# Decayed attention and two expanding layers on one core: four edits to the opening and to the order of the second products

## The reference, cut to what matters

```python
for t in range(S):                       # attention: 4 batches, 8 heads, 768 tokens, 48 wide
    state = alpha[:, :, t, :, None] * state + np.einsum('bhd,bhe->bhde', k[:, :, t], v[:, :, t])
    y[:, :, t] = np.einsum('bhd,bhde->bhe', q[:, :, t], state)
x = y.transpose(0, 2, 1, 3).reshape(3072, 384)
h = x @ w_in;   g = h * np.tanh(softplus(h));  x = g @ w_out      # first layer, 384 -> 2048 -> 384
h = x @ w_in2;  g = h * np.cos(h);             out = g @ w_out2   # second layer, the same shape
```

## Time and profile before

| | us |
|---|---|
| three runs | 902.21, 902.39, 904.98 |
| median | 902.39 |
| the profiled execution | 904.68 |
| its span, first to last instruction | 902.6 |
| PE busy (matmuls) | 887.0 (98% of the span) |
| DVE, ACT, POOL busy | 402.9, 410.4, 361.2 |
| mean granted TensorE clock | 0.994 |

### The profile page before, as it was taken

One profiled execution on the slowest core, in us unless ns is written; L12 is line 12 of the kernel. 1 busy time (PEld: TensorE's weight loads), 2 busy tenths in 40 slices (PEclk: granted clock), 3 DMA queues, 4 the chain that ended last, 5 costly groups with the idle time before them and its releaser, 6 DMA issues.

```text
span 902.6 us, 13960 instructions
## 1 busy us (share of the span) xinstructions
PE 887.0 (98%) x5536; PEld 729.0 (81%) x5536; DVE 402.9 (45%) x625; ACT 410.4 (45%) x702; POOL 361.2 (40%) x281
## 2 busy tenths in 40 slices
PE   7799999999999999999999999999999999999997
PEld 6588888888888888888888788888888888888885
DVE  8664432222223322210021666665666575666653
ACT  3344332223223232322354756565665565665654
POOL 3576344444443345442256333332323232323332
PEclk9899999999999999999999999999999999999999
DMA  8535321112112311210032300200200200200000
GB/s 218 167 98 161 98 74 39 39 39 75 39 39 54 95 41 39 74 30 1 36 123 91 101 2 1 70 1 1 70 1 1 71 0 1 71 1 1 35 1 36
DMA packets 17153, 48.13 MB, mean 53 GB/s; under 512 B 2752, under 2 KB 2752, under 8 KB 17088
## 3 DMA queue, kind: packets, MB, share of 16 engines
q1 hardware_dynamic: 17088, 47.23, 17.8%
HBM read 37.79 MB, written 9.44 MB: 52 GB/s over the span
## 4 chain that ended last, share of the span: by engine, by line
PE 52%; issue 29%; POOL 14%; DVE 2%; DMA 1%; ACT 1%; POOLq 0%; ACTq 0%; SPq 0%; DVEq 0%
PE bank L413 22%; PE bank L433 22%; POOL g_lo L762 14%; PE bank L341 3%; PE bank L362 2%; PE bank L369 1%; PE bank L374 1%; PE bank L335 1%; PE bank L385 1%; DMA shared<-mid 1%; DVE growth L604 0%; DVE suffix L593 0%; DMA shared<-aqk_in 0%; DVE w_lo L651 0%; DVE probs L625 0%
## 5 line engine op out<-in xcount | busy, mean ns | idle before, releaser
L762 POOL TENSOR_TENSOR g_lo<-g,g_hi 128x512 fp32r<-128x512 f32 x192 | 263.3, 1372 | 484.3 <-ACT g_hi L506 484.3
L433 PE MATMUL bank<-g_hi,w_hi 128*128 128x512 f32 x576 | 226.9, 394 | 0.3 <-DVE x_out L664 0.3
L433 PE MATMUL bank<-g_lo,w_hi 128*128 128x512 f32 x576 | 224.6, 390 | 0.6 <-POOL g_lo L762 0.6
L433 PE MATMUL bank<-g_hi,w_lo 128*128 128x512 f32 x576 | 224.3, 389 | 0.0
L506 ACT ACTIVATE g_hi<-g 128x512 fp32r<-128x512 f32 x192 | 120.6, 628 | 145.1 <-PE bank L433 143.5
L413 PE MATMUL bank<-x_hi,w_hi 128*128 128x512 f32 x576 | 163.0, 391 | 4.7 <-POOL w_lo L754 3.6
L413 PE MATMUL bank<-x_hi,w_lo 128*128 128x512 f32 x576 | 162.4, 390 | 0.0
L413 PE MATMUL bank<-x_lo,w_hi 128*128 128x512 f32 x576 | 162.4, 390 | 0.0
L413 PEld LDWEIGHTS bank<-x_hi,w_hi 128*128 128x128 f32 x576 | 108.1, 188 | 28.4 <-issue 4.0
L433 PEld LDWEIGHTS bank<-g_hi,w_hi 128*128 128x128 f32 x576 | 108.1, 188 | 25.2 <-DVE x_out L664 0.7
L433 PEld LDWEIGHTS bank<-g_lo,w_hi 128*128 128x128 f32 x576 | 108.1, 188 | 24.7 <-POOL g_lo L762 1.9
(11 more groups left out here) (69 smaller groups left out, 594.8 us busy)
## 6 DMA issues: line engine op xcount, KB each, us to landing
w_raw<-w_in SPq DMA_DIRECT2D x32, 384.0 KB, 3.5
shared<-aqk_in SPq DMA_DIRECT2D x44, 192.0 KB, 3.6
v_sb<-v_in SPq DMA_DIRECT2D x24, 256.0 KB, 4.5
shared<-aqk_in SPq DMA_DIRECT2D x48, 96.8 KB, 3.9
mid<-x_out SPq DMA_DIRECT2D x6, 768.0 KB, 5.1
shared<-mid SPq DMA_DIRECT2D x6, 768.0 KB, 5.7
out<-x_out SPq DMA_DIRECT2D x5, 768.0 KB, 4.0
out<-x_out SPq DMA_DIRECT2D x3, 256.0 KB, 2.4
```

The source lines that it names most:

```text
L433: mm = nc.tensor.matmul(acc[m][:, :], wp[:, f, cols], gp[:, tile % GB, :], start=(f == 0 and n == 0), stop=(f == FT - 1 and n == 2))
L762: nc.gpsimd.tensor_tensor(g_lo[:, tile % GB, :], g[:, tile % GB, :], g_hi[:, tile % GB, :].bitcast(F32), ALU.subtract).then_inc(glo_ready, 1)
```

## The change

Five things are changed. ACT and POOL split piece 2 earlier. The masked scores of chunks 1 and 3 go to a buffer of their own (the unused third parts of `x_out` and `g`), and `mask` of chunks 2 and 3 waits for one `values` less. `add_state` of chunks 1 to 3 moves from DVE's opening into step 2, behind `mask(4)`. Second products of slices above 0 take the three matmuls with `g_lo` last; for the very last tile each bank reports by itself when it is done (`last_done`), and ACT takes the last tile's absolute value (`fold`) ahead of `g_part` of the tile before it. Seven `warm` matmuls are added.

```diff
+        def probs_of(c, i):
+            if c in (1, 3):
+                return (x_out[:, 2, :], g[:, 2, :])[i].rearrange("p (a t) -> p a t", a=PAIRS)
+            return probs[:, i, :, :]
...
-                for m in range(KT):
-                    if f == 0 and j > 0:
+                parts = ((w_hi, g_hi), (w_lo, g_hi), (w_hi, g_lo))
+                order = [(m, n) for m in range(KT) for n in range(3)]
+                if f > 0:
+                    order = [(m, n) for m in range(KT) for n in range(2)] + [(m, 2) for m in range(KT)]
+                for i, (m, n) in enumerate(order):
+                    if f == 0 and j > 0 and n == 0:
...
-                        if m == 0 and gp is g_lo:
-                            pe.wait_ge(glo_ready, tile + 1)
...
+                    if (m, n) == (0, 2):
+                        pe.wait_ge(glo_ready, tile + 1)
+                    wp, gp = parts[n]
...
+                    if tile == 2 * TILES - 1 and n == 2:
+                        mm.then_inc(last_done, 1)
+                    elif i == len(order) - 1:
+                        mm.then_inc(out_done, 1)
...
             scores(0)
-            warm(4)
+            warm(8)
             scores(1)
+            warm(3)
             values(0, -1)
...
             def take_acc(j):
-                act.wait_ge(out_done, FT * (j + 1))
+                last = j == 2 * BLOCKS - 1
+                if not last:
+                    act.wait_ge(out_done, FT * (j + 1))
                 if j > 0:
                     act.wait_ge(stored, 16 * j)
                 for m in (0, 2):
+                    if last:
+                        act.wait_ge(last_done, m + 1)
...
+                if s == 2 * TILES:
+                    fold(s - 1)
                 if alive(s - 2) and s - 2 >= TILES:
                     g_part(s - 2)
                 if alive(s - 1) and s - 1 >= TILES:
+                    if s < 2 * TILES:
+                        fold(s - 1)
                     cosine(s - 1)
...
             split_w(1)
+            split_w(2)
             keep_x_hi(3)
-            split_w(2)
             split_w(3)
...
             def mask(c):
-                if c >= 1:
-                    dve.wait_ge(y_done, c)
+                if c >= 2:
+                    dve.wait_ge(y_done, c if c >= BATCH else c - 1)
...
                     mask(c)
+                if s == 2:
+                    for c in range(1, BATCH):
+                        add_state(c)
...
-            for c in range(BATCH):
-                add_state(c)
+            add_state(0)
             split_w(3)
...
             split_w(0)
+            split_w(2)
             prepare(4)
-            split_w(2)
```

More of the change, by code:

```diff
@@ L206, in program @@
         out_done = sem("out_done")
+        last_done = sem("last_done")
         acc_act = sem("acc_act")
@@ L369, in values @@
                         nc.tensor.matmul(turn[32 * n:32 * n + 32, k * P:(k + 1) * P],
-                                         v_sb[:, c % 3, h, at:at + 32], probs[:, h % 2, h // 2, :],
+                                         v_sb[:, c % 3, h, at:at + 32], probs_of(c, h % 2)[:, h // 2, :],
                                          start=(c < BATCH and k == 0), stop=True, skip_group_check=True)
@@ L375, in values @@
                                               v_sb[:, c % 3, 2 * n + i, 32 - 32 * i:64 - 32 * i],
-                                              probs[:, i, n, :], start=False, stop=True, skip_group_check=True)
+                                              probs_of(c, i)[:, n, :], start=False, stop=True, skip_group_check=True)
                 mm.then_inc(y_done, 1)
@@ L428, in second_product @@
                             pe.wait_ge(acc_act, 2 * (j - 1) + m // 2 + 1)
-                    cols = slice(DM + m * P, DM + (m + 1) * P)
-                    for n, (wp, gp) in enumerate(((w_hi, g_hi), (w_lo, g_hi), (w_hi, g_lo))):
-                        if m == 0 and gp is g_lo:
-                            pe.wait_ge(glo_ready, tile + 1)
-                        mm = nc.tensor.matmul(acc[m][:, :], wp[:, f, cols], gp[:, tile % GB, :],
-                                              start=(f == 0 and n == 0), stop=(f == FT - 1 and n == 2))
-                mm.then_inc(out_done, 1)
+                    if (m, n) == (0, 2):
+                        pe.wait_ge(glo_ready, tile + 1)
+                    wp, gp = parts[n]
+                    mm = nc.tensor.matmul(acc[m][:, :], wp[:, f, DM + m * P:DM + (m + 1) * P], gp[:, tile % GB, :],
+                                          start=(f == 0 and n == 0), stop=(f == FT - 1 and n == 2))
+                    if tile == 2 * TILES - 1 and n == 2:
+                        mm.then_inc(last_done, 1)
+                    elif i == len(order) - 1:
+                        mm.then_inc(out_done, 1)
             def step(s):
@@ L521, in turns, with fold @@
                                      scale=1.0 / TWO_PI).then_inc(u_ready, 1)
-            def cosine(tile):
+            def fold(tile):
                 n = tile - TILES
@@ L527, in cosine @@
                 nc.scalar.activation(here, here, ACT.Abs).then_inc(abs_ready, 1)
+            def cosine(tile):
+                n = tile - TILES
+                here = t[:, tile % 3, :]
                 act.wait_ge(abs_ready, n + 1)
@@ L620, in mask @@
             def mask(c):
-                if c >= 1:
-                    dve.wait_ge(y_done, c)
+                if c >= 2:
+                    dve.wait_ge(y_done, c if c >= BATCH else c - 1)
                 for i in range(2):
                     dve.wait_ge(scores_done, 2 * c + i + 1)
-                    nc.vector.tensor_tensor(probs[:, i, :, :], score_banks(c)[i][:, :].rearrange(
+                    nc.vector.tensor_tensor(probs_of(c, i), score_banks(c)[i][:, :].rearrange(
                         "s (p t) -> s p t", p=PAIRS), causal[:, None, :].to_broadcast([P, PAIRS, P]),
@@ L660, in take_acc @@
             def take_acc(j):
-                dve.wait_ge(out_done, FT * (j + 1))
+                if j == 2 * BLOCKS - 1:
+                    dve.wait_ge(last_done, 2)
+                else:
+                    dve.wait_ge(out_done, FT * (j + 1))
                 if j > 0:
```

## The result

| | before | after |
|---|---|---|
| median, runs timed together (6 and 6) | 902.3 | 897.39 |
| lowest to highest | 901.61 to 904.98 | 897.13 to 897.96 |
| ratio of times, 95% interval | | 0.9942 [0.9929, 0.9954] |
| the profiled execution | 904.68 | 897.42 |
| its span | 902.63 | 895.39 |

The kernel is 4.9 us faster by the medians; 7.0 were forecast (902.39 to 895.3). By the two profiled executions it is 7.3 faster, where the sum said 8.2.

A forecast was written before the change was run, and what follows sets the result against it. PE sets the pace in the middle, so only its waits in the opening and last 15 us could pay: 6.2 + 1.55 + 0.45 = 8.2, giving medians of 894.2 to 896.5, forecast 895.3; range 893.3 to 897.7.

The forecast's parts named there:

- the rival that came true: Step 3: DVE loses its turn to POOL and `first_product(4)` stalls by 1.4, giving 896.7; chance 0.12.
- the lost turn: Step 3: POOL, not DVE, goes next when both wait, delaying `first_product(4)` by about 1.4; chance 0.12.
- a clock term: Opening, tile 2 and `scores(4)`: 6.43 falls to 3.7 at the full PE clock, a gain of 2.7.
- the step from tile 3 to tile 4 still about 6.5: Sign in the opening: the time between the first products of tiles 3 and 4 stays about 6.5 us.
- Tile 3 was forecast at 36.64: Opening: first product of tile 3 starts at 36.64 against 42.83, 6.2 us earlier; bounds 3.5 and 6.6.
- The end's 1.55 and 0.45: Last tiles: PE's waits for `g_hi` and `g_lo` go, 1.55; `last_done` starts copies and the first store 0.45 earlier.
- the rival "slower": Second products: more bank changes cost PE time, 8.1 at 15 ns each, 905.5 or more from 20 ns; chance 0.03.
- By the row DVE goes next … no stall: Step 3: DVE's split starts by F3 + 4.4, `add_state(4)` ends by F3 + 6.1, so `first_product(4)` doesn't wait.
- the forecast's slack was 0.4: Step 3: the margin before `first_product(4)` would wait for DVE, which spoke for DVE losing its turn; chance 0.12.
- If all runs lose the 2.7 of the clock alike: Opening: with the clock loss equal in all runs the median becomes 894.2; otherwise it comes to 896.5.
- The warm matmuls: "nothing": Opening, before `scores(1)` and `values(0)`: seven idle matmuls fit PE's waits, worth nothing, at worst a loss of 0.1.
- 0.54 was forecast: Opening, F0 (tile 0's first product): 0.54 of `mask(3)`'s 0.93 wait is gained, 26.88 against 27.42; bounds 0 and 0.93.

The follow-up runs named there:

- e0_after: The changed kernel, unchanged, run again beside the kernel before: 897.19, ratio 0.9929 against before.
- u_end: The changed kernel with the end as before (`g_lo` interleaved, no `last_done`, `fold` in its old place): 899.6, ratio 0.9952 against before.
- e2_act: e1 with piece 2 in ACT's old order (`keep_x_hi(3)` ahead of it) and POOL's new one: 896.26, ratio 0.9917 against before.
- u_warm: The changed kernel without the seven added `warm` matmuls: 898.01, ratio 0.9931 against before.
- u_probs: The changed kernel with one buffer of masked scores again: 896.59, ratio 0.9918 against before.
- u_state: The changed kernel with the six state additions back in DVE's opening, ahead of `split_w(3)`: 899.52, ratio 0.9961 against before.
- b_split: The kernel before with only the early split of piece 2 on ACT and POOL: 901.03, ratio 0.9965 against before.
- e1: The changed kernel with DVE's split of piece 5 moved behind `add_state(4)` and `keep_x_lo(4)`: 895.94, ratio 0.9916 against before.
- b_warm: The kernel before with 12 idle matmuls in PE's wait ahead of tile 2: 901.44, ratio 0.9976 against before.
- the second set: Five rounds of follow-up runs undoing parts of the change one by one; before's median there 903.71, the unchanged changed kernel's 897.19.
- c0_before: The kernel before, unchanged, as a control with a second profile: 903.54, ratio 0.9998 against before.
- e4_bank: e1 with a bank of its own for tile 1, so its first product needn't wait for `mish` of tile 0: 895.67, ratio 0.9911 against before.
- u_split: The changed kernel with piece 2's split in the order of before on ACT and POOL: 900.16, ratio 0.9957 against before.

## Why the prediction was right, and where it was not

The measured 897.39 lies in the stated range (893.3 to 897.7), but above the forecast's own 894.0 to 896.8. The range had room for the rival that came true; the forecast by itself missed, by the lost turn and by a clock term that was sized too large. Of the signs that were named, only "the step from tile 3 to tile 4 still about 6.5" failed.

**The opening up to tile 3 and the end: right by their terms.** Tile 3 was forecast at 36.64 and started there. That it fits to the hundredth is luck: in e0_after it starts at 36.26, and counted from the start of the first mask it came 6.42 earlier (22.75 after it instead of 29.17), where 6.2 were forecast. The end's 1.55 and 0.45 came to 1.46 and 0.42, and u_end, which undoes both, loses 1.83 in its own tail and 2.4 in the median. The middle is untouched, and there is no price on changing banks: the rival "slower" is out, since a steady step takes 4.08 in before, in after and in u_end, which keeps the old order. (By its own terms that rival comes to 902.39 - 8.2 + 10.8 = 905.0 at 20 ns, not to 905.5; nothing hangs on it.)

**The step that failed: "By the row DVE goes next … no stall".** It was worked out from one meeting, in which DVE had waited for POOL's `g_lo` and then went first. At 40.33 DVE waited for a `g_lo` as well, and POOL went first. The trace of before had this outcome too, ten us ahead of the row that was read (POOL's and DVE's timelines):

```profile
52.42 1.19 POOL L776 TENSOR_TENSOR shared<-shared,growth 112x512 f32<-112x512 f32 x1 [1.23 <-DVE growth L604]
53.03 2.19 DVE L651 TENSOR_TENSOR w_lo<-w_raw,w_hi 128x768 fp32r<-128x768 f32 x1 [0.76 <-ACT w_hi L471]
53.57 0.84 POOL L783 TENSOR_TENSOR state<-state,suffix 112x384 f32<-112x384 f32 x1
```

DVE asked at 53.03, during POOL's queries, and was done at 55.22: POOL's decay, until 54.41, went first, and 0.81 was left for the split. The rule cited there (SBUF — State Buffer, section "SBUF: two separate sides", of the Trainium skill) holds in both cases: while POOL's instruction ran, DVE's split of two inputs in SBUF stood still, and the additions, which read a bank, ran on at 0.38 each beside POOL's `g_lo`. The rule leaves open who is next, and so did the rows of before, read together. At 57 to 63 us DVE's split went ahead of POOL's in all 14 traces (in e2_act behind a whole `g_lo`, 2.17); those around 40 us went POOL's way in after, e0_after, u_end, u_warm and u_probs, and in u_state and b_split one at 35.5 did. What decides it stays open: no run tried it, and the kind of work doesn't, since at both places POOL had a `g_lo` under way and a split next. The price given to the rival, 1.4, was right (1.35, and 1.35 back in e1), its chance of 0.12 too low: the forecast's slack was 0.4 against a whole instruction of POOL, 1.85. Had the step been taken as even, the middle would have been nearer to 896.

**The size that was off: the clock.** "If all runs lose the 2.7 of the clock alike": they don't. The level alone is worth 2.1 in the median (b_warm), and in a second profile of before it cost 1.55. With 2.1 for the clock instead of 2.7, 1.35 + 0.14 off for the lost turn and what follows it, and 0.12 off for the end, the sum of 8.2 becomes 6.0. Measured were 4.9 in the first comparison and 6.5 in the second set; before's own median lies between 902.3 and 903.9 in the four comparisons, so this bill can't be drawn up closer than to about 1 us. Of the 2.3 by which the profiled execution of before lay above its fellows, the clock explains a part (0.8 between the groups of clocks, over the 30 runs), the load at steps 87 and 88 up to 0.62, which is in that profile and not in all others; the rest isn't settled.

**The warm matmuls: "nothing" is not shown wrong in the median, but it isn't safe.** Without them three of five runs show a lower mean clock and take 1.3 more than the other two; no trace shows where. What one profile shows of the level doesn't hold in all runs: the first profile of before has the lower level from 14.98 to 18.39, in the first `values`, and the second, c0_before, doesn't.

**The second buffer of masked scores: its term was right at F0, and worth nothing at the end.** F0 came 0.56 earlier where 0.54 was forecast; counted from the start of the first mask it is 0.79 against the first profile of before, which had the lower level there, 0.63 against the second, and 0.66 by u_probs. But tile 4 stood behind DVE and POOL, which had their own pace, so it was spent on a longer wait there. The same happened to the two attempts at more: what e2_act and e4_bank win before tile 3 they lose in step 5, to POOL's queries.

**What carried the gain** is the two orders together, and the end (2.4, u_end). The early split alone is worth 2.9 (b_split) and leaves tile 3 waiting for piece 3; the moved additions take that wait away (2.3, u_state) and make the new one in step 3. The split of piece 5 belongs behind them: e1_late5, 1.3 to 1.5 below after, beats both kernels.

## What to carry to other kernels

Where two engines share a port, price a meeting with at least one whole further instruction of the other (it was two at 32.01 in u_split), look at several meetings in the trace before taking a turn for granted, and put what a third engine waits for ahead of the instruction that may lose its turn. A gain in an early stage is worth what arrives behind the next engine that paces the work: follow it to the next wait on that engine, not to the next start on PE. A loss of clock behind an idle stretch differs from run to run, so take its price from more than one execution, or fill the stretch with idle matmuls and measure.

## What the runs showed of the hardware that had not been expected

- POOL went on to its next instruction while DVE waited: 3.38 us for a split of 0.95 in after. In u_split it went on to two, 4.02 us.
- The lower level came behind a named wait of only 2.07 us (u_state); behind one of 1.41 (b_split) PE stayed at 1.00. Behind the wait of 3.6 in before it stood for 6.8 us in one profile and 3.4 in another, and cost 2.7 and 1.55.
- Twelve idle matmuls kept the level up through a wait that PE could not shorten, for 2.1 us. Without seven small ones in the opening, three of five runs were 1.3 us slower than the other two, at a lower mean clock.
